# Limiting the 24 indirect gathers of combine weights, behind the last expert tile, to two in flight

## The reference

```python
x = attention_with_gates(q, k, v, i_gate, f_gate, o_gate)     # -> (3072, 320)

# first mixture: each token goes to one expert
e   = argmax(x @ w_gate);  x = prob[e] * (relu(x @ w1[e]) @ w2[e])

# second mixture: 32 slots, four of each expert, each a weighted mean over all tokens
logits     = x @ phi                                          # (3072, 32)
d          = softmax(logits, axis=0);  slot_in = d.T @ x      # (32, 320)
slot_out   = relu(slot_in[4e:4e+4] @ v1[e]) @ v2[e]           # for each expert e
c          = softmax(logits, axis=1)                          # combine weights
out        = c @ slot_out                                     # (3072, 320)
```

## Time and profile before

| | us |
|---|---|
| median of 3 runs | 645.27 (642.56 to 646.26) |
| the profiled execution: its time | 648.21 |
| the profiled execution: span from first to last instruction | 646.5 |
| PE busy / PE weight loads busy | 557.5 / 478.8 |
| DVE / ACT / POOL busy | 376.2 / 251.8 / 313.7 |
| mean granted clock of PE | 0.914 |
| DMA: bytes, mean rate | 91.63 MB, 142 GB/s |

### The profile page before, as it was taken

The page is one execution under the profiler, slowest core; times in us unless marked ns, Lnnn a source line. Parts: engine busy times, 40 slices in busy tenths (PEclk is TensorE's granted clock), DMA queues, the critical chain, the costliest instruction groups (busy, mean ns, idle before and its releaser), DMA issues.

```text
span 646.5 us, 12037 instructions
## 1 busy us (share of the span) xinstructions
PE 557.5 (86%) x3643; PEld 478.8 (74%) x3644; DVE 376.2 (58%) x656; ACT 251.8 (39%) x606; POOL 313.7 (49%) x241
## 2 busy tenths in 40 slices
PE   2899998999999317999999999999999999886583
PEld 1798997998898316898888888989889889822022
DVE  6488886798689693644737767474654334330013
ACT  3776765866574521223323233233233233210003
POOL 3455553655364444554899668593570000107600
PEclk9998996998699555999999999999999999979588
DMA  8999999999992002335451505050501800199047
GB/s 115 160 198 223 199 236 223 207 245 229 208 244 53 20 2 71 97 109 171 134 165 47 201 22 191 21 191 21 185 12 39 330 12 1 33 342 286 19 163 244
DMA packets 149689, 91.63 MB, mean 142 GB/s; under 512 B 108128, under 2 KB 142944, under 8 KB 145568
## 3 DMA queue, kind: packets, MB, share of 16 engines
q1 hardware_dynamic: 138784, 80.58, 51.4%
q0 software_dynamic: 2256, 5.48, 3.4%
q10 hardware_dynamic: 8624, 5.26, 2.6%
HBM read 78.07 MB, written 8.47 MB: 134 GB/s over the span
## 4 chain that ended last, share of the span: by engine, by line
PE 46%; SPq 15%; DVE 13%; DMA 12%; issue 8%; POOL 3%; ACT 2%; DVEq 0%; POOLq 0%; ACTq 0%
DMA ys<-x_tokens,slot_i 7%; PE bank L1288 5%; PE bank L1290 5%; PE bank L1289 5%; SPq L347 4%; SPq L348 4%; PE bank L1271 4%; PE bank L1417 3%; PE bank L1273 3%; PE bank L1272 3%; PE bank L1299 3%; PE bank L1193 2%; SPq L361 2%; DVE gates L1002 2%; PE bank L1313 2%
## 5 line engine op out<-in xcount | busy, mean ns | idle before, releaser
L556 POOL TENSOR_TENSOR W_low<-W,W_high 128x3072 fp32r<-128x3072 f32 (+1 forms) x14 | 87.2, 6228 | 7.2 <-ACT W_high L694 6.3
L1288 PE MATMUL bank<-W_high,h_high 128*128 x248 | 79.3, 320 | 1.5 <-DVE h_low L1027 1.4
L740 ACT ACTIVATE h_high<-bank 128x512 fp32r<-128x512 f32 x62 | 33.7, 595 | 119.6 <-PE bank L1299 115.4
L593 POOL TENSOR_TENSOR W_high<-W,ones 128x3072 fp32r<-128x3072 f32 (+1 forms) x12 | 58.6, 4883 | 37.5 <-PE bank L1290 37.5
L1289 PE MATMUL bank<-W_high,h_low 128*128 x248 | 76.6, 309 | 0.0
L1290 PE MATMUL bank<-W_low,h_high 128*128 x248 | 76.5, 309 | 0.0
L623 ACT ACTIVATE arena<-arena 128x128 f32<-128x128 f32 x192 | 60.6, 391 | 17.4 <-DMA arena<-log_decays 12.8
L1271 PE MATMUL bank<-W_high,x_high 128*128 x124 | 52.9, 427 | 5.7 <-DVE x_high L1010 2.5
L983 DVE TENSOR_TENSOR yc<-bank,slot_gate 128x320 f32<-128x320 f32 x31 | 15.2, 492 | 72.9 <-PE bank L1290 72.9
L1015 DVE TENSOR_SCALAR hb<-bank 128x512 f32<-128x512 f32 x31 | 21.3, 689 | 56.8 <-PE bank L1275 56.8
L1002 DVE TENSOR_TENSOR gates<-gates,rmx (+1 forms) x31 | 52.0, 1681 | 0.0
(11 more groups left out here) (235 smaller groups left out, 1268.9 us busy)
## 6 DMA issues: line engine op xcount, KB each, us to landing
W<-in_moe_w_rows_dram SPq DMA_DIRECT2D x13, 1280.0 KB, 8.4
W<-in_moe_w_main_dram SPq DMA_DIRECT2D x13, 1024.0 KB, 5.2
arena<-log_decays SPq DMA_DIRECT2D x24, 512.0 KB, 5.2
W<-in_moe_w_rest_dram SPq DMA_DIRECT2D x21, 256.0 KB, 5.9
xs<-ys ACTq DMA_DIRECT2D x29, 160.0 KB
ys<-in_q_dram SPq DMA_DIRECT2D x24, 160.0 KB, 5.1
ys<-in_k_dram SPq DMA_DIRECT2D x24, 160.0 KB, 5.7
ys<-in_v_dram SPq DMA_DIRECT2D x24, 160.0 KB, 5.2
```

The source lines that it names most:

```text
L556: g.tensor_tensor(W_low[:, w], W[:, w], W_high[:, columns(e % 2, part_)].bitcast(F32), ALU.subtract).then_inc(w_split[part_], 1)
L593: g.tensor_tensor(W_high[:, columns(e % 2, part_)], w, ones[:, 0:1].broadcast_to(list(w.shape)), ALU.mult).then_inc(high_ready, 1)
L1288: mm(dst, h_high[:, kk, :], high, start=(kk == 0), stop=False)
```

## The change

The one semaphore `c_back` becomes two. Gather t adds to number t % 2, and from the third gather on POOL first waits until gather t - 2 has landed. The two places that wait for all 24, on DVE and on PE, wait for both semaphores, 12 gathers on each. Nothing else is changed: no instruction stands in another place, and the same 24 gathers move the same bytes.

```diff
-        c_max, c_stored, c_back, c_sums = sem("c_max"), sem("c_stored"), sem("c_back"), sem("c_sums")
+        c_max, c_stored, c_sums = sem("c_max"), sem("c_stored"), sem("c_sums")
+        c_back = [sem(f"c_back{n}") for n in range(2)]
...
             pool.wait_ge(c_stored, 16 * (TILES - 1))
             for t in range(NT):
+                if t >= 2:
+                    pool.wait_ge(c_back[t % 2], 16 * (t // 2))
                 g.indirect_dma_start(ctok[:, t, :], None, c_dram,
-                                     bass.IndirectOffsetOnAxis(ap=pos_i[:, t:t + 1], axis=0)).then_inc(c_back, 16)
+                                     bass.IndirectOffsetOnAxis(ap=pos_i[:, t:t + 1], axis=0)).then_inc(c_back[t % 2], 16)
...
                 if q == 1:
-                    dve.wait_ge(c_back, 16 * NT)
+                    for n in range(2):
+                        dve.wait_ge(c_back[n], 16 * (NT // 2))
...
             def transpose_combine():
-                pe.wait_ge(c_back, 16 * NT)
+                for n in range(2):
+                    pe.wait_ge(c_back[n], 16 * (NT // 2))
```

## The result

The median of four runs is 659.3 us (657.74 to 660.51), against 645.37 for the kernel before beside it (four runs, 642.56 to 646.26). The ratio is **1.0217 [1.0182, 1.0253]**, 13.9 us slower. The prediction said slower, with 0.73; but 659.3 is 4.8 us above its 654.5 and 1.8 us outside its range. The profiled execution took 660.51 us at a span of 658.7 and a mean granted clock of 0.907.

A forecast was written before the change was run, and what follows sets the result against it. It took the last stage as bound by weights, then PE's slow `soft1(1)`, with gathers off the chain. The median 645.3 plus 9.2 us for a longer slow phase gave 654.5 us, range 646.0 to 657.5.

The forecast's parts named there:

- The waits bite under load: On POOL, the new waits leave about 5 us idle before gather 2 and again before gather 4.
- The term for gather 23: Last gather starts at 620.95 and is seen landed at 623.4 instead of 613.1, 10.3 us later.
- Rival 1: Short queue cures PE's slow issue, but earlier weights slow the gathers; last lands 628.7, +6.8, 652.1 us; chance 0.30.
- working theory: In the last stage PE issues slowly while gathers land, so the slow phase lasts 10.3 us longer too.
- the +9.2 us: Slow phase ends at 626.2, then 8.4 us of weights; `soft2(1)` starts at 634.6 instead of 625.38.
- The slack of 8.8 us: Gathers land at 613.09, and nothing else needs them until PE ends `soft1(1)` at 621.86.
- Semaphores at nothing: One more wait each on DVE and PE costs nothing, below 0.1 us each.
- Rival 2: PE's slow phase is unrelated to the gathers and ends at 616 as now; 646.8 us; chance 0.15.
- Rival 3: PE is cured and loaded gathers take turns with the weights, all landing at 614; 637.9 us; chance 0.10.
- Rival 4: POOL's waits stop nothing, because landings are faster than its 1.25 us of issue; given no chance of its own.

The follow-up runs named there:

- c_before: The kernel before with only PE's expert number loaded by a bounded load, the control: 638.09 us; again on a third chip 649.24 us.
- c_after: The change on the kernel before with PE's expert number loaded by a bounded load: 653.38 us; again on a third chip 657.29 us.
- late2: `c_after` with PE's transposes moved behind the spread, DVE's sum and ACT's copies also behind quad 1: 646.71 us, kernel before 649.49.
- quiet2: `c_after` with SP holding the weights of experts 5 to 7 until all gathers landed: gathers took 33.5 us, first start to last landing.
- two_sems: `c_before` with two alternating semaphores but no wait on POOL, all 24 gathers in flight: cost nothing, last landing not timed separately.
- late4_hold: `c_before` with four gathers in flight, their users behind quad 1, and expert 4's weights held until combine weights are stored: 0.9866 of the kernel before.
- half: `c_before` with only 12 gathers, the other 12 tiles' combine weights set to 1: last landing 34.7 us behind the tile.
- pad64: `c_before` with 64 semaphore increments near the start of PE's program: 1.0040 of the kernel before, 3.5 us slower.

## Why the prediction was right or wrong

- **The waits bite under load: right.** It gave about 5 us ahead of gathers 2 and 4; 4.57 and 5.73 were measured. The term for gather 23, seen landed at 623.4 and so 10.3 us later, was too low: it was 13.9 us in these two traces, counted behind the tile (DVE's sum at 64.2 against 50.2). It was the term for the case in which the last weights go out late. They went out at 596.05 and kept the DMA engines full beyond 606. From gather 2 to gather 4 took 7.9 us where the sum had 6.5, and from 4 to 6 took 6.3 where it had 3.6. Rival 1 had this step right: DVE's sum 628.7 - 581.86 = 46.8 us behind gather 0, measured 632.11 - 585.57 = 46.5.
- **The step that failed: "I take it as the working theory that PE issues slowly while these gathers land."** It fails even with 24 in flight: in `c_before` all 48 loads of `soft1(1)` went from 593.96 to 603 while gathers landed one behind the other. With two in flight, PE crawled in none of five traces (the change, `c_after`, `c_after_b`, `late2`, `quiet2`). So the +9.2 us, built from a crawl until 626.2, a `soft_done` behind it and 8.4 us of weights, did not happen: `soft_done` came at 28 us behind the tile, and the end was set by the gathers' own landing. That is what rival 1 describes, and its `soft2(1)` at 69.4 behind the tile was measured at 69.1. The argument against it was that PE was slow between 600 and 612 with at most two in flight. That shows only that a crawl which has begun goes on with few in flight, not that two begin one. That two in flight are what keeps the crawl away isn't shown either: wherever it came, it set in 24.3 to 30.8 us behind the tile, with `soft2(0)` still under way, and in `c_before` and `two_sems`, with 24 in flight, that layer was through by 27.0. With two in flight it was through by 29 too, so that PE may only have been done in time.
- **The slack of 8.8 us: right for that trace, not for the kernel.** It was read off one execution in which PE crawled until 616. In an execution without the crawl, PE waits for the gathers already, and the delay reaches the end in full: 13.1 of 13.3. This is the likelier reason that the sums of the forecast and of rival 1 end at 652 to 655 and the runs at 659. The profiled execution's 648.21, above every one of the timed runs, was a hint of it. That the runs of before had mostly no crawl is the reading that fits the 13.9; it isn't shown for them, as no trace of theirs exists. The groups agree with it: between the first group's chip, whose control has no crawl in its trace, and the third's, whose control has one, `c_after`, which crawls on neither, differs by 3.9 us (653.38 and 657.29) and the control by 11.2 (638.09 and 649.24); the 7.3 us between these are near the 8 of the crawl. The other reading, 7.2 us of stage and the 5.1 us ahead of it, isn't excluded.
- **Semaphores at nothing: right** (`two_sems`). **Rival 2** fell with the early SP line. **Rival 3** fell by the loaded gathers, 5.5 to 8.3 us each. **Rival 4** had nothing, as said.
- **The 5.1 us ahead of the stage stay open.** The tile's end is at 567.9, 561.4 and 566.4 us in the three traces of the change, at 562.8, 559.6, 559.9 and 561.8 in those of the kernel before and its control, and at 558.6 and 560.2 in `late2` and `quiet2`, which also have two in flight. It was at 567.7 in `late4_hold`, so the late ends are not tied to two in flight.

What starts the crawl stays open too. It was in all traces with 24 in flight but two (`c_before`, `two_sems`), in the one with eight and in `half`, and it ends 2.6 to 4.5 us behind the last landing, with 12 gathers as with 24. That ties its end to the gathers; it does not give the cause. In six of its eight traces it lies in `soft2(0)` alone. In those of before and `pad64` PE's last load of `soft2(0)` is at 593.96 and 607.25 us, and the crawl goes on in `soft1(1)`; yet SP's line still waits, until 615.88 and 617.99, when the crawl is over. Why the signal comes so late there isn't known.

## What to carry to other kernels

A limit on transfers in flight costs (time of one under the load of that moment, less depth x issue time) for each round of the queue. Depth 8 was free here, 4 made the last landing 7 us later and 2 made it 13, and almost all of it fell where large loads of another queue were running. Slack that is read from one trace is the slack of that execution. If its own time stands at the edge of the timed runs, or if a phase in it has "issue" as its only reason, price the change also for a kernel without that phase. And where a small result is late, first look for what needs it before the end: six transposes and a sum moved behind quad 1 gave back all that the change had taken.

## What the runs showed that was not expected

- PE can issue at a third to a twentieth of its rate with no wait in the program, for 11 to 27 us, while gathers of POOL are queued, and the same program can be without it on another chip: 3 weight loads in 6 us in `c_before_b`, 64 in the 6 us from 582 in `c_before`. Its beat is one load or one matmul in 0.70 us. The stage is 8 us longer with it (84.7 against 76.7).
- PE's granted clock falls in both kinds of execution: to the lower level, 0.50, in the crawl, and to a mean of 0.60 over the 22 us in which PE was all but idle behind the gathers in the change.
- A gather of 16 KB takes 2.3 us from its start to its landing on nearly idle DMA engines, and 5.5 to 8.3 us when another queue has them full.
- 128 semaphore increments near the start of PE's program made it 10.7 us slower (1.0168 [1.0128, 1.0208]), all of that ahead of the last stage.
